# Gate and value projections by a seven-product scheme, in two passes over the tokens

## What is computed

```python
for t in range(S):                                     # 8 heads of 64, S = 768
    state = gamma * state + outer(k[t], v[t])
    y[t] = scale * (q[t] @ state)
x = y reshaped to (3072, 512)
xn = x / sqrt(mean(x * x) + 1e-6) * rms_g
a = silu(xn @ w_gate) * (xn @ w_val)                   # 512 -> 1536, twice
x2 = a @ w_out                                         # 1536 -> 512
h = x2 @ w_in                                          # 512 -> 1024
solu = h * softmax(h)
out = layernorm(solu) * g_ln @ w_out2                  # 1024 -> 512
```

## Time and profile before

| what | us |
|---|---|
| median of 3 runs | 1037.94 (1037.87 to 1038.93) |
| the profiled execution | 1038.56 |
| its span, first to last instruction | 1036.8 |
| PE busy | 1013.7 |
| DVE / ACT / POOL busy | 461.4 / 431.4 / 89.7 |
| first matmul of a gate group starts at | 50.43 |
| first matmul of stage C starts at | 550.55 |

### The profile page before, as it was taken

The page is one execution under the profiler, slowest core; times in us unless marked ns, Lnnn a source line. Parts: engine busy times, 40 slices in busy tenths (PEclk is TensorE's granted clock), DMA queues, the critical chain, the costliest instruction groups (busy, mean ns, idle before and its releaser), DMA issues.

```text
span 1036.8 us, 15804 instructions
## 1 busy us (share of the span) xinstructions
PE 1013.7 (98%) x5656; PEld 886.8 (86%) x5656; DVE 461.4 (45%) x874; ACT 431.4 (42%) x776; POOL 89.7 (9%) x101
## 2 busy tenths in 40 slices
PE   6799999999999999999999999999999999999998
PEld 3489999999999999999998888888888888888886
DVE  3847636356352473524324643243253253254243
ACT  3445334243332432323214474364364364265255
POOL 5331110111101110100001000000000000000000
PEclk9899999999999999999999999999999999999999
DMA  7664331533315334322135211012012012012000
GB/s 234 211 218 143 112 113 48 167 117 106 109 54 159 117 96 126 107 85 87 66 123 187 74 62 61 24 54 85 0 61 101 0 61 94 7 61 92 11 21 31
DMA packets 75657, 95.53 MB, mean 92 GB/s; under 512 B 7248, under 2 KB 59728, under 8 KB 75600
## 3 DMA queue, kind: packets, MB, share of 16 engines
q1 hardware_dynamic: 69840, 79.06, 23.4%
q0 software_dynamic: 3744, 13.63, 3.8%
q10 hardware_dynamic: 2016, 2.04, 0.7%
HBM read 64.04 MB, written 30.67 MB: 91 GB/s over the span
## 4 chain that ended last, share of the span: by engine, by line
PE 93%; DVE 2%; ACT 2%; issue 1%; ACTq 1%; DMA 1%; SPq 0%; DVEq 0%
PE psum L285 28%; PE psum L286 28%; PE psum L287 28%; PE psum L542 3%; PE psum L532 2%; PE psum L620 2%; PE psum L523 2%; PE psum L509 1%; DMA v_buf<-v_rows 1%; PE psum L559 1%; ACTq L340 0%; ACT L819 0%; ACTq L346 0%; DVE w_gv_lo L953 0%; DVE solu L1054 0%
## 5 line engine op out<-in xcount | busy, mean ns | idle before, releaser
L285 PE MATMUL psum<-xn_hi,w_gv_hi 128*128 128x384 f32 x768 | 265.8, 346 | 0.8 <-issue 0.8
L286 PE MATMUL psum<-xn_lo,w_gv_hi 128*128 128x384 f32 x768 | 257.2, 335 | 0.0
L287 PE MATMUL psum<-xn_hi,w_gv_lo 128*128 128x384 f32 x768 | 257.2, 335 | 0.0
L775 ACT ACTIVATE silu<-psum 128x384 f32<-128x384 f32 x96 | 47.1, 491 | 277.8 <-PE psum L287 277.8
L285 PEld LDWEIGHTS psum<-xn_hi,w_gv_hi 128*128 128x128 f32 x768 | 144.9, 189 | 4.2 <-issue 3.2
L286 PEld LDWEIGHTS psum<-xn_lo,w_gv_hi 128*128 128x128 f32 x768 | 144.8, 188 | 0.9
L287 PEld LDWEIGHTS psum<-xn_hi,w_gv_lo 128*128 128x128 f32 x768 | 144.4, 188 | 0.0
L1015 DVE TENSOR_TENSOR act_buf<-psum,silu 128x384 f32<-128x384 f32 x96 | 53.5, 558 | 189.8 <-PE psum L287 109.4
L285 PE MATMUL psum<-act_hi,w_out_hi 128*128 128x512 f32 x288 | 114.2, 397 | 0.0
L287 PE MATMUL psum<-act_hi,w_out_lo 128*128 128x512 f32 x288 | 112.3, 390 | 0.0
L286 PE MATMUL psum<-act_lo,w_out_hi 128*128 128x512 f32 x288 | 112.3, 390 | 0.0
(11 more groups left out here) (82 smaller groups left out, 1438.3 us busy)
## 6 DMA issues: line engine op xcount, KB each, us to landing
act_dram<-act_buf SPq DMA_DIRECT2D x96, 192.0 KB, 1.9
act_raw<-act_dram SPq DMA_DIRECT2D x72, 256.0 KB, 2.7
w_raw<-weights POOLq DMA_DIRECT2D x26, 512.0 KB, 4.6
kq_buf<-k_t SPq DMA_DIRECT2D x32, 192.0 KB, 2.7
kq_buf<-q_t SPq DMA_DIRECT2D x64, 96.0 KB, 2.9
out<-out_buf SPq DMA_DIRECT2D x24, 256.0 KB, 2.0
k_buf<-k_rows SPq DMA_DIRECT2D x29, 192.0 KB, 2.8
v_buf<-v_rows SPq DMA_DIRECT2D x29, 192.0 KB, 3.1
```

Source lines behind the costliest of these rows:

```text
L285: pe.matmul(dst, w_hi, m_hi, start=start, stop=False)
L286: pe.matmul(dst, w_hi, m_lo, start=False, stop=False)
L287: return pe.matmul(dst, w_lo, m_hi, start=False, stop=stop)
L775: act.activation(silu[:, f % 2, :], psum[:, GATE[f % 2], 0:TB], ACT.Silu).then_inc(silu_ready, 1)
```

## The change

**Seven products instead of eight.** For a chunk of features f and the 768 tokens of a batch, gate and value together are a 2 x 2 block product: weights (gate, value) by two halves of the inputs, tokens by two halves of the inputs and two halves of the tokens. The kernel before makes it of 8 block products (each 2 slices times 3 matmuls of 384 columns). The changed kernel makes it of 7 (P1, P7, P6, P2, P5, P4, P3 in this order; `PRODUCTS`), with sums and differences of blocks. One f of one batch is called a quad here, and one of its seven places a point.

**Sums ahead.** Of the weights, GpSimd makes four sums for each f (`sum_gv`, 128 x 256 each), and hi and lo are made of 7 blocks (`gv_high`, `gv_low`, two parts) instead of 4. Of the tokens, VectorE makes three differences for each batch (`make_t`, 128 x 768) and GpSimd one (`make_t3`), and hi and lo are made of 7 blocks (`operand_high`, `operand_low`, 128 x 768 each) instead of 4.

**Sums behind, in PSUM.** Three banks hold a quad: ScalarE copies P1 from bank PX to PY ahead of P6, and P7 out of PV (`p7_buf`); VectorE adds PY after P6 and `p7_buf` into PV (L1203), ahead of P5; and adds them again after P5 (`c22`, L1207), ahead of P3. VectorE multiplies the first half of the tokens (L1212), GpSimd the second (`second_act`). PE waits for `xy_copied` at P6, for `u3_ready` at P5 and for `c22_ready` at P3.

**Two passes.** The weights of 12 chunks as 7 blocks don't fit beside the attention. So there are 8 windows: windows 0 to 3 are batches 0 to 3 with chunks 0 to 4 (`FA = 5`: 35 points each), windows 4 to 7 the same batches with chunks 5 to 11 (49 points each). The normalised tokens are stored to `x_dram` (`store_xn`) and loaded again for the second pass (`load_x`). The steps of batches 1, 2, 3 stand in windows 0, 1, 2, at points 3 to 20 of 35 (`ENTRIES`), two of them at each of 8 points (`DOUBLES`), with no product between the two. All 24 steps of batch 0, and the normalisation of both its halves, stand ahead of window 0. The windows are written out, without a loop.

```diff
-    STEP_AT = steps_at(range(4, 9), range(10, 23, 2), range(23, 26), range(27, 48, 2))
...
-    LEFT = 5
...
+    PRODUCTS, HK = 7, KC // 2
...
+    FA = 5
+    FB = FC - FA
...
+    DOUBLES = (6, 8, 10, 12, 14, 16, 18, 19)
+    FIRST_STEP, LAST_STEP = 3, 20
+    ENTRIES = [g for g in range(FIRST_STEP, LAST_STEP + 1) for _ in range(2 if g in DOUBLES else 1)]
...
+    SUM_AT, ROOT_AT, INVERT_AT, SCALE_AT = 14, 14, 15, (16, 17)
...
+        def windows(attention_step, point):
+
+            for m in range(WINDOWS):
+                for j, f in enumerate(features(m)):
+                    for i in range(PRODUCTS):
+                        if m < B - 1:
+                            for ch in STEPS.get(j * PRODUCTS + i, ()):
+                                attention_step(m + 1, ch)
+                        point(m, j, f, i)
...
+            def point(m, j, f, i):
+                n = first_quad(m) + j
+                if m < B - 1 and j * PRODUCTS + i == LAST_STEP + 2:
+                    sum_squares(2 * (m + 1) + 1)
+                if j == 0:
+                    pe.wait_ge(xo_lo_ready, PRODUCTS * m + CONVERTED[i])
...
+                if i == P1:
+                    at_least(pe, silu1_ready, n)
+                elif i == P7:
+                    at_least(pe, act1_ready, n)
+                elif i == P6:
+                    pe.wait_ge(xy_copied, n + 1)
+                elif i == P5:
+                    pe.wait_ge(u3_ready, n + 1)
+                elif i == P3:
+                    pe.wait_ge(c22_ready, n + 1)
+                dst = psum[:, {P1: PX, P2: PX, P7: PV, P4: PV}.get(i, PY), 0:TB]
+                hi, lo = slot(f)
+                for kc in range(HK):
...
                 if ch > 0 and run_of(ch - 1)[3] < KVS:
                     update_state(b, ch - 1)
-                if not is_first(b) and ch + 1 < BC:
+                if b > 0 and ch + 1 < BC:
                     kq_low(b, ch + 1)
...
+                if HC < ch < BC and ch % HC == 1:
+                    add_squares(b, (ch - 1) // HC - 1)
+                if ch == BC:
+                    add_squares(b, RUNS - 1)
+                if ch == INVERT_AT:
+                    invert_rms(2 * b, 0)
+                    invert_rms(2 * b, 1)
+                if ch in SCALE_AT:
+                    scale_x(2 * b, SCALE_AT.index(ch))
```

800 lines of the change are left out of this document (480 added, 320 removed).

## The result

The changed kernel takes 1091.39 us (median of four runs, 1088.20 to 1092.81) against 1037.90 us for the kernel before (1036.94 to 1038.93): a ratio of 1.0508, 95% interval 1.0491 to 1.0526. The forecast was 1071 with a range of 1030 to 1096. The sign and the range held, and the main mechanism with them (PE waits for VectorE in the windows with the attention); the time is 20 us above the forecast and near the top of the range, and this part asks where the 20 us come from. The profiled execution took 1090.09 us.

The account below looks back on a forecast made before the run. PE, busy 98% of the span, was taken as the bound. Start 76.5, weights' lo parts 1.5, PE's work 438.8, attention-window waits 61.2, rest 4, stage C 1 + 486.3: span 1069.3, forecast 1071 us, range 1030 to 1096.

Parts of the forecast that it names:

- The sign: Whole kernel: the change makes it slower, 3.2% by the forecast; chance of slower 0.77.
- the main mechanism: Windows 0 to 2: PE waits for VectorE's chain of mask, state update and `kq_lo`, 15.5 us a window.

## What to carry to other kernels

A scheme that saves one product in eight moves its cost to the engines that make its sums. Ask in each stage whether those have the time, and not only whether their total fits: VectorE, at 45% of the span before and 72% of these windows after, made PE wait in the windows with the attention, while the same change gains some 24 us in windows 3 to 7 (33 quads of 48 matmuls at 0.1734 us are 274.7 us; these windows took 250.5). Where two engines take turns in one in-order queue, cutting a dependence gives back only the difference to the next thing in the queue; count the work per step on both engines first. And a wait of PE has to be priced with the clock behind it: 0.7 to 0.9 of the lost speed was lost time at the two places where the same instructions ran at both clocks, even ahead of a wait of over 3.5 us.

## What I had not expected of the hardware

- The granted clock went to 0.50 for some 3.4 us at a time, once for 7 (172 to 179), at idle times of 1 to 3 us, in windows that were over 80% busy as a whole. Fourteen matmuls of filling at each of two places per window kept it at 1.00 through windows 1 and 2.
- GpSimd took 1.83 to 1.86 us for a difference of 768 columns where no difference of VectorE's started beside it, 2.56 to 2.63 beside VectorE's first difference; VectorE takes 0.95. It took 1.23 to 1.32 us for 256 columns of the weights' sums beside VectorE's work; the earlier trace rows has 1.0 us for 384 columns of 64 partitions.
- How often VectorE is held by GpSimd depended on the phase of the two, and the phase changed with the order: fourteen of 72 `kq_lo` over 1.0 us before, two after, with the same 64 instructions of `q_dec` beside them.
